# Fused attention and two mixture-of-experts layers on one core: the copies, low parts, ranks, slot gates and weight chunks between expert 7 and the fourth tile of the second layer change places

## The chip, the core and the metric

The kernel runs on one core of one Trainium2 chip. The time is the device time of one execution in microseconds; one program for each engine runs from the first attention block to the last scatter of the output. Shown are the median of three runs and one execution taken by the profiler. Engines are named as the profile names them: PE is TensorE, ACT ScalarE, DVE VectorE, POOL GpSimd, and SP the engine that issues the large loads.

## The reference

Windowed attention with sink tokens is followed by two mixture-of-experts layers. The first takes two experts for each token (noisy routing), the second one expert:

```python
def _moe2_ref(x, modality_id, w_gate, modality_bias, w1, w2):
    logits = x @ w_gate + modality_bias[modality_id]
    e_idx = np.argmax(logits, axis=1)
    probs = softmax(logits)                      # over the 8 experts
    gate_w = probs[np.arange(N), e_idx]
    for e in range(E):                           # E = 8, D = 512, F = 1024, N = 1536
        mask = e_idx == e
        h = np.maximum(x[mask] @ w1[e], 0.0)
        out[mask] = gate_w[mask, None] * (h @ w2[e])
```

The input x of this layer is the output of the first one. All values are float32; the kernel keeps that precision by splitting each operand of a product into a high part (rounded) and a low part (the rest), and adding three products: high by high, high by low, low by high.

## The kernel before

The program is written out by hand for each engine, and an engine executes its instructions in the written order. Semaphores alone tie the engines together, so the order in the text is the order on the chip. The first layer goes through eight experts, numbered 0 to 7. Expert 7 (`last` in the text) is its last. While it is computed, the router of the second layer already works on what the other experts have produced.

**What the second layer is made of.** The tokens are sorted by their expert and cut into tiles of 128 rows. The expert that most tokens of the first eight token blocks choose is called popular; its first two tiles (tiles 0 and 1) are made of tokens that are settled early, so that PE can begin while the rest of the routing is still under way. A tile t goes through these steps, which are small functions in the text:

- POOL `gather(t)` fetches its 128 rows from memory (L730); PE `tx(t)` turns them (L1320); ACT `x_high(t)` copies the turned rows as the high part (L1698) and DVE `x_low(t)` writes the low part (L2410).
- PE `first(t, half)` is the first product, in two halves of twelve 512-column matmuls: eight with the high part of the rows (L1339, L1340), four with the low part (L1344). ACT `relu(t, half)` copies the result (L1704).
- PE `th(t, half)` turns the hidden rows (L1354); ACT `h_high` (L1709) and DVE `h_low` (L2416) make their two parts.
- PE `second(t)` is the second product, again two halves of twelve matmuls (L1367, L1368, then L1371). DVE `y_copy(t)` scales the rows by their gates (L2424), and POOL scatters them.

From tile 4 on a loop runs these steps in a fixed pattern (`step`), in which `first` of tile t and `second` of tile t - 1 alternate.

**Weights.** A chunk is 128 by 2048 values, 1024 KB; an expert has four (0 and 1 for the first product, 2 and 3 for the second). SP loads it, ACT makes the high part, DVE the low part. Those of the popular expert are `popular_high(c)` (L1689) and `popular_low(c)` (L2402). Those of the expert that comes second in order are loaded by SP (L503 to L516) into `raw`, and converted by ACT and DVE in `second_weights` (L1446 and L1817); ACT's two calls of it stand between `x_high(2)` and `relu(2, 0)`, and behind `x_high(3)`. SP can load them only when it knows which expert it is: DVE's `expert_order()` (L2098 to L2106) says so.

**Routing of the second layer.** DVE `pick` finds each token's expert, PE `ranks(1)` counts (L956 to L960), DVE `second_places` (L2074 to L2090) finds each token's place, `second_hots` (L2093) and PE `codes2` (L977) make the list of rows that is gathered from tile 2 on, and `second_sources` (L2120 to L2126) writes it. ACT's exponential (L1766), DVE `chosen_gate` and POOL `coded_gates` (L709 to L718) lead to PE `slot_gates` (L1393) and DVE `slot_gates` (L2198 to L2201), the gates by slot, which every `y_copy` needs. `tile_owners` and `fresh_tiles` say which expert owns which tile.

**Expert 7.** PE's last product ends in `yT`; ACT `y1_copy(last, 3)` (L1592) takes its last part out of PSUM, and PE `last_logits(3)` (L1136) waits for that. PE `back(last, k)` (L1199) turns its rows back, four times, ACT `last_scale(k)` (L1624) scales them, and POOL scatters them. DVE `last_share` (L2333 to L2337) prepares its part in the router, which PE `last_to_tokens` (L1146) adds.

## Time and profile before

| | us |
|---|---|
| median of three runs | 679.68 |
| lowest and highest of the three | 679.19 and 680.46 |
| profiled execution | 680.44 |
| its span in the trace | 678.7 |
| PE busy | 640.8 (94%) |
| DVE busy | 328.6 (48%) |
| ACT busy | 275.7 (41%) |

The change lies between about 467 us, when PE ends the last product of expert 7, and 530.8 us, when the fourth tile's second product is still to come and the loop begins. Before and behind that stretch no instruction moves.

### The profile page before, as it was taken

How to read it: one execution, taken by the hardware profiler on the slowest of the kernel's cores; microseconds unless marked ns; L12 is line 12 of the kernel's file. 1: busy time of each engine (PE TensorE's matmuls, PEld its weight loads, DVE VectorE, ACT ScalarE, POOL GpSimd, SP SyncE). 2: the span in 40 equal slices, each digit the busy share in tenths (PEclk: the TensorE clock that was granted, in tenths of full speed). 3: DMA queues.
4: the chain of work that ended last, by engine and by line, in shares of the span. 5: the costliest groups of instructions: out<-in, count | busy, mean ns of one | idle time of the engine just before them, and what ended most of it. 6: DMA issues, size and time to landing. Idle time of an engine off the chain costs nothing.

```text
span 678.7 us, 11243 instructions
## 1 busy us (share of the span) xinstructions
PE 640.8 (94%) x3866; PEld 581.7 (86%) x3867; DVE 328.6 (48%) x681; ACT 275.7 (41%) x529; POOL 188.1 (28%) x199
## 2 busy tenths in 40 slices
PE   7989999899999999999999999998989999999981
PEld 6989999898999999999999998987767888788861
DVE  4466646586465527264452724566767222442220
ACT  5678866443344234243433523234516122522110
POOL 2500100127361633516153331101643122121010
PEclk9999999999999999999999999998989999999996
DMA  7878721354594546646364611515559311001000
GB/s 213 273 256 250 262 85 58 103 210 130 178 235 149 101 140 155 188 144 171 103 134 149 155 20 20 153 62 177 150 168 340 113 44 50 20 31 48 15 32 11
DMA packets 51089, 89.84 MB, mean 132 GB/s; under 512 B 7919, under 2 KB 14063, under 8 KB 51040
## 3 DMA queue, kind: packets, MB, share of 16 engines
q1 hardware_dynamic: 41872, 69.21, 30.8%
q0 software_dynamic: 9168, 19.97, 13.5%
q8 instruction: 31, 0.51, 0.3%
q14 instruction: 18, 0.15, 0.1%
HBM read 73.13 MB, written 17.02 MB: 133 GB/s over the span
## 4 chain that ended last, share of the span: by engine, by line
PE 80%; DVE 7%; DMA 4%; issue 3%; ACT 2%; SPq 1%; POOL 0%; ACTq 0%; DVEq 0%; POOLq 0%
PE banks L1058 6%; PE banks L1057 6%; PE banks L1076 6%; PE banks L996 5%; PE banks L997 5%; PE banks L999 5%; PE banks L801 5%; PE banks L829 4%; PE banks L1344 4%; PE banks L1339 4%; PE banks L1340 4%; PE banks L1367 3%; PE banks L1371 3%; PE banks L1368 3%; PE banks L813 2%
## 5 line engine op out<-in xcount | busy, mean ns | idle before, releaser
L1821 DVE TENSOR_TENSOR split<-stage,split 128x2048 fp32r<-128x2048 f32 x32 | 73.3, 2290 | 42.2 <-ACT split L1451 42.1
L996 PE MATMUL banks<-xTs,split 128*128 128x416 f32 (+1 forms) x256 | 88.7, 351 | 1.6 <-issue 1.6
L997 PE MATMUL banks<-xTs,split 128*128 128x416 f32 (+1 forms) x256 | 86.4, 342 | 0.0
L648 POOL DMA_INDIRECT x_moe<-rows,dst_idx x25 | 50.3, 2013 | 114.9 <-DVE rows L2271 112.9
L1057 PE MATMUL banks<-hTs,split 128*128 128x416 f32 x224 | 79.9, 357 | 0.0
L1058 PE MATMUL banks<-hTs,split 128*128 128x416 f32 x224 | 78.6, 351 | 0.0
L1586 ACT ACTIVATE hTs<-banks 128x416 fp32r<-128x416 f32 x56 | 29.0, 518 | 85.4 <-PE banks L999 85.4
L1451 ACT ACTIVATE split<-stage 128x2048 fp32r<-128x2048 f32 x32 | 60.9, 1908 | 0.5 <-DMA stage<-w1a 0.5
L1709 ACT ACTIVATE hTs<-banks 128x512 fp32r<-128x512 f32 x28 | 16.5, 598 | 105.1 <-PE banks L1354 105.1
L999 PE MATMUL banks<-xTs,split 128*128 128x416 f32 (+1 forms) x256 | 56.2, 341 | 0.0
L801 PE MATMUL banks<-k_sb,q_sb 128*128 128x260 f32 (+2 forms) x192 | 49.5, 384 | 3.4 <-DMA k_sb<-k_w 2.0
L1831 DVE CUSTOM_DVE_ANT_0 negs<-banks,masks 128x260 f32<-128x260 f32 (+2 forms) x96 | 35.0, 402 | 35.9 <-PE banks L801 34.5
L996 PEld LDWEIGHTS banks<-xTs,split 128*128 128x128 f32 x256 | 48.1, 188 | 2.5 <-issue 2.2
L1984 DVE SCALAR_TENSOR_TENSOR hTs<-banks,hTs 128x416 fp32r<-128x416 f32 x56 | 32.8, 587 | 35.8 <-ACT hTs L1586 35.7
L746 POOL DMA_INDIRECT out<-rows,dst x14 | 14.2, 1015 | 128.0 <-DVE rows L2424 118.5
L1464 ACT ACTIVATE probs<-negs,negmax 128x260 f32<-128x260 f32 (+2 forms) x96 | 46.1, 484 | 7.9 <-DVE negmax L1831 7.8
L1367 PE MATMUL banks<-split,hTs 128*128 (+1 forms) x112 | 45.7, 408 | 3.6 <-DVE rows L2424 1.8
L1339 PE MATMUL banks<-split,xTs 128*128 (+1 forms) x112 | 45.4, 405 | 3.6 <-issue 2.0
L2245 DVE TENSOR_TENSOR xTs<-banks,xTs 128x512 fp32r<-128x512 f32 (+1 forms) x28 | 16.6, 592 | 66.4 <-ACT xTs L1555 66.3
L997 PEld LDWEIGHTS banks<-xTs,split 128*128 128x128 f32 x256 | 48.2, 188 | 0.3
L1076 PE MATMUL banks<-hTs,split 128*128 128x416 f32 x224 | 48.0, 356 | 0.0
L999 PEld LDWEIGHTS banks<-xTs,split 128*128 128x128 f32 x256 | 46.3, 188 | 0.4
(371 smaller groups left out, 1313.6 us busy)
## 6 DMA issues: line engine op xcount, KB each, us to landing
stage<-w1a SPq DMA_DIRECT2D x16, 1024.0 KB, 7.3
stage<-w2a SPq DMA_DIRECT2D x16, 1024.0 KB, 5.5
k_sb<-k_w SPq DMA_DIRECT2D x12, 520.0 KB, 4.9
raw<-w1b SPq DMA_DIRECT2D x4, 1024.0 KB, 6.1
raw<-w2b SPq DMA_DIRECT2D x4, 1024.0 KB, 8.8
q_sb<-q_t SPq DMA_DIRECT2D x24, 128.0 KB, 4.1
x_attention<-rows SPq DMA_DIRECT2D x12, 256.0 KB, 6.0
split<-x_moe SPq DMA_DIRECT2D x12, 256.0 KB, 3.7
```

What stands on the lines that cost most here:

```text
L648: pool.indirect_dma_start(out=x_dram[1], out_offset=rows_at(dst_idx[0], early_dst, e, k), in_=y_lines(e, k), in_offset=None, compute_op=AL ...
L801: mm = pe.matmul(S[:, j % 2, h, 0:n], q_sb[:, b, pair, h, :], k_sb[:, b, pair, 0:n], start=True, stop=True)
L996: pe.matmul(psum, piece(slot, 0, o + c * FH), xTs[:, 0, c, 0:cols], start=(c == 0), stop=False)
L997: pe.matmul(psum, piece(slot, 1, o + c * FH), xTs[:, 0, c, 0:cols], start=False, stop=False)
L999: mm = pe.matmul(psum, piece(slot, 0, o + c * FH), xTs[:, 1, c, 0:cols], start=False, stop=(c == DC - 1))
L1057: pe.matmul(psum, piece(e % 2, 0, o), hTs[:, 0, c, 0:cols], start=(c == 0), stop=False)
L1058: pe.matmul(psum, piece(e % 2, 1, o), hTs[:, 0, c, 0:cols], start=False, stop=False)
L1076: mm = pe.matmul(psum, piece(e % 2, 0, DC * F + c * D + d * P), hTs[:, 1, c, 0:cols], start=False, stop=(c == FC - 1))
L1339: pe.matmul(psH[:, half, :], xTs2[:, 0, c, :], weights(slot, 0, o), start=(c == 0), stop=False)
L1367: pe.matmul(psY, hTs2[:, 0, c, :], weights(slot, 0, o), start=(c == 0), stop=False)
L1451: act.activation(split_chunk(e % 2, 0, c), staged_chunk(e % 2, c), ACT.Copy).then_inc(high_done[c], 1)
L1821: dve.tensor_tensor(split_chunk(e % 2, 1, c), staged_chunk(e % 2, c), split_chunk(e % 2, 0, c).bitcast(F32), ALU.subtract).then_inc(low_do ...
```

## The change

It changes the written order on four engines, and takes out one wait; no instruction with a result is added or taken away.

- ACT: `popular_high(0)` goes behind `y1_copy(last, 3)`. `relu(0, 0)` goes ahead of `last_scale(3)`, the exponential ahead of `relu(0, 1)`, `popular_high(3)` behind `x_high(1)`, and `parted_tiles` behind `h_high(0, 0)`.
- DVE: `popular_low(0)` goes behind `last_share`, `x_low(0)` and `popular_low(1)` ahead of `pick`. `chosen_gate` and `popular_low(2)` go ahead of `x_low(1)` and `second_places`. `h_low(0, 0)` and `popular_low(3)` go ahead of `second_sources`; `slot_gates` and `y_copy(0)` ahead of `expert_order`; `tile_owners` and `fresh_tiles` behind `h_low(1, 1)`; `y_copy(1)` ahead of the second expert's low parts.
- PE: `first(0, 0)` goes ahead of `back(last, 3)`, `ranks(1)` behind `tx(1)`. `codes2` moves into the middle of `second(0)`. The wait for all four `last_scale` moves from `first(0, 1)` to `th(0, 0)`; `first(0, 1)` waits for the first of them only. `th(2, 0)` goes ahead of `first(3, 0)`: the call of `step(3)` is written out for that.
- SP: ahead of the loads of the second expert's weights the wait for the gather of tile 2 is gone.

```diff
--- before.py
+++ after.py
@@ -508,7 +508,6 @@
             experts = sp.value_load(used[0:1, 1, 1:2], min_val=1, max_val=E)
             e = sp.value_load(order[0:1, 1:2], min_val=0, max_val=E - 1)
             sp.wait_ge(last_added, 1)
-            sp.wait_ge(gathered[0], 32)
             for c in range(CHUNKS):
                 if c == CHUNKS - 1:
                     sp.wait_ge(all_scattered, 1)
@@ -1358,8 +1357,11 @@
                     if not isinstance(t, int) or t > 0:
                         pe.wait_ge(y_copied, t)
                     for half in range(2):
-                        if isinstance(t, int) and t == 1 and half == 1:
-                            tx(2, 0, 2)
+                        if isinstance(t, int) and half == 1:
+                            if t == 0:
+                                codes2()
+                            elif t == 1:
+                                tx(2, 0, 2)
                         pe.wait_ge(low_done[2 + half], e + (E + 1))
                         pe.wait_ge(h_high_done, t * 2 + (half + 1))
                         for c in range(half * 4, half * 4 + 4):
@@ -1396,16 +1398,16 @@
 
                 tx(0, 0, 1)
                 back(last, 2, banks[:, 3, :])
+                first(0, 0, 0, 1)
                 back(last, 3, banks[:, 4, :])
-                first(0, 0, 0, 1)
-                ranks(1)
-                pe.wait_ge(scaled1, nth_sub(E, 0))
+                pe.wait_ge(scaled1, nth_sub(last, 0) + 1)
                 first(0, 1, 0, 1)
                 tx(1, 1, 1)
+                ranks(1)
                 first(1, 0, 0, 1)
+                pe.wait_ge(scaled1, nth_sub(E, 0))
                 th(0, 0)
                 first(1, 1, 0, 1)
-                codes2()
                 th(0, 1)
                 second(0, 0, 1)
                 slot_gates()
@@ -1413,11 +1415,17 @@
                 th(1, 1)
                 second(1, 0, 1)
                 pe.wait_ge(fresh_ready[1], 1)
-                e, slot = expert(2)
-                first(2, 0, e, slot)
-                first(2, 1, e, slot)
+                e2, slot2 = expert(2)
+                first(2, 0, e2, slot2)
+                first(2, 1, e2, slot2)
                 tx(3, 1, 2)
-                step(3, 1, 3)
+                th(2, 0)
+                e3, slot3 = expert(3)
+                first(3, 0, e3, slot3)
+                first(3, 1, e3, slot3)
+                th(2, 1)
+                tx(4, 0, 3)
+                second(2, e2, slot2)
                 with pe.Fori(2, sure // 2 - 1) as r:
                     step(r * 2, 0, r + 1)
                     step(r * 2 + 1, 1, r + 2)
@@ -1681,7 +1689,6 @@
                 y1_copy(last, 2)
                 x2_high(11)
                 turned_copy(2)
-                popular_high(0)
                 y1_copy(last, 3)
 
             def popular_high(c):
@@ -1752,22 +1759,23 @@
                             act.wait_ge(pe_route, 7)
                         high_part(1, c)
 
+                popular_high(0)
                 popular_high(1)
                 last_scale(0)
                 last_scale(1)
                 x_high(0)
                 last_scale(2)
+                relu(0, 0)
                 last_scale(3)
                 popular_high(2)
-                relu(0, 0)
-                popular_high(3)
-                relu(0, 1)
                 act.wait_ge(act_route, 6)
                 act.activation(rc[:], rb[:], ACT.Exp).then_inc(act_route, 1)
+                relu(0, 1)
                 x_high(1)
-                parted_tiles()
+                popular_high(3)
                 relu(1, 0)
                 h_high(0, 0)
+                parted_tiles()
                 relu(1, 1)
                 h_high(0, 1)
                 h_high(1, 0)
@@ -2456,36 +2464,36 @@
                         dve.wait_ge(high_done[c], E + 2)
                         low_part(1, c)
 
-                popular_low(0)
                 popular_first()
                 last_share()
-                popular_low(1)
+                popular_low(0)
                 late_scores()
                 all_scores()
+                x_low(0)
+                popular_low(1)
                 pick(noisy, 0, chosen[:], done_key)
                 dve.sem_inc(dve_route, 1)
                 link(dve.tensor_tensor(rb[:], noisy[:], over_e(top[:, 0, :]), ALU.subtract))
                 dve.sem_inc(act_route, 1)
-                x_low(0)
+                chosen_gate()
+                popular_low(2)
+                x_low(1)
                 second_places()
-                x_low(1)
-                chosen_gate()
                 second_hots()
-                popular_low(2)
-                second_sources()
                 h_low(0, 0)
                 popular_low(3)
+                second_sources()
                 h_low(0, 1)
+                slot_gates()
+                y_copy(0, 0, 0)
                 expert_order()
+                h_low(1, 0)
+                h_low(1, 1)
                 tile_owners()
                 fresh_tiles()
-                slot_gates()
-                y_copy(0, 0, 0)
-                h_low(1, 0)
-                h_low(1, 1)
                 x_low(2)
+                y_copy(1, 1, 0)
                 second_weights((0, 1))
-                y_copy(1, 1, 0)
                 x_low(3)
                 second_weights((2, 3))
                 next_weights(2)
```

On ACT at the end of expert 7 and in tile 0, before (`stage` are the staged weight chunks of the popular expert, `yT` the last part of expert 7's product, `raw` the scaled rows of expert 7):

```order
L1618 ACTIVATE rows<-banks 16x512
L1689 ACTIVATE split<-stage 128x2048
L1592 ACTIVATE yT<-banks 128x416
L1689 ACTIVATE split<-stage 128x2048
L1624 ACTIVATE raw<-banks,sub_gate 128x512 x2
L1698 ACTIVATE xTs<-banks 128x512
L1624 ACTIVATE raw<-banks,sub_gate 128x512 x2
L1689 ACTIVATE split<-stage 128x2048
L1704 ACTIVATE rows<-banks 128x512
L1689 ACTIVATE split<-stage 128x2048
L1704 ACTIVATE rows<-banks 128x512
L1766 ACTIVATE rc<-rb 128x96
```

and with the change, where the lines carry other numbers (L1592 is L1600, L1689 is L1696):

```order
L1626 ACTIVATE rows<-banks 16x512
L1600 ACTIVATE yT<-banks 128x416
L1696 ACTIVATE split<-stage 128x2048 x2
L1632 ACTIVATE raw<-banks,sub_gate 128x512 x2
L1705 ACTIVATE xTs<-banks 128x512
L1632 ACTIVATE raw<-banks,sub_gate 128x512
L1711 ACTIVATE rows<-banks 128x512
L1632 ACTIVATE raw<-banks,sub_gate 128x512
L1696 ACTIVATE split<-stage 128x2048
L1772 ACTIVATE rc<-rb 128x96
L1711 ACTIVATE rows<-banks 128x512
L1705 ACTIVATE xTs<-banks 128x512
```

The copy of `yT` no longer has the first weight chunk ahead of it, and the fourth weight chunk has gone behind the copy of tile 1's turned rows (`xTs`).

On DVE, from the low part of the hidden rows of tile 0 on, before (`used` and `order` are what the loads of the second expert wait for; the last row here is the first of `tile_owners`):

```order
L2402 TENSOR_TENSOR split<-stage,split 128x2048
L2416 TENSOR_TENSOR hTs<-banks,hTs 128x512
L2098 TENSOR_REDUCE noise_sb<-pair_up_to 128x2
L2099 CAST used<-noise_sb 128x1
L2101 TENSOR_TENSOR noise_sb<-pair,iota_row 128x8
L2102 SCALAR_TENSOR_TENSOR pair_sq<-iota_row,pair_up_to 128x64
L2103 TENSOR_TENSOR pair_sq<-pair_sq,noise_sb 128x64
L2104 TENSOR_REDUCE order_f<-pair_sq 128x8
L2105 CAST order<-order_f 128x7
L2110 SCALAR_TENSOR_TENSOR shared<-pair_up_to,iota_row 128x168
```

and with the change (`slot_gate` are the gates by slot, the row behind it is `y_copy(0)`):

```order
L2424 TENSOR_TENSOR hTs<-banks,hTs 128x512
L2206 COPY shared<-banks 128x63
L2208 TENSOR_TENSOR shared<-shared 128x21
L2209 TENSOR_TENSOR slot_gate<-shared 128x21
L2432 TENSOR_SCALAR rows<-banks,slot_gate 128x512
L2106 TENSOR_REDUCE noise_sb<-pair_up_to 128x2
L2107 CAST used<-noise_sb 128x1
L2109 TENSOR_TENSOR noise_sb<-pair,iota_row 128x8
L2110 SCALAR_TENSOR_TENSOR pair_sq<-iota_row,pair_up_to 128x64
L2111 TENSOR_TENSOR pair_sq<-pair_sq,noise_sb 128x64
L2112 TENSOR_REDUCE order_f<-pair_sq 128x8
L2113 CAST order<-order_f 128x7
```

Ahead of the order of the experts three instructions of the slot gates and the copy of tile 0's result have moved.

## Rows read from the trace of the kernel before

**Rows 1.** Windows: us, busy of PE, PEld, DVE, ACT, POOL, PEclk, DMA share, GB/s.
```profile
467.10:470.40 3.30, 1.50 (x15) 1.41 (x14) 1.13 (x1) 2.70 (x3) 2.00 (x2) 1.00 0.98 341
470.50:477.20 6.70, 6.14 (x73) 5.71 (x73) 6.13 (x16) 3.45 (x5) 3.11 (x1) 0.50 0.63 211
...
501.20:504.50 3.30, 1.48 (x10) 1.11 (x9) 2.94 (x11) 1.08 (x2) 0.02 (x1) 1.00 0.70 208
504.70:508.00 3.30, 3.30 (x9) 2.52 (x8) 0.05 (x1) 0.00 (x0) 0.80 (x1) 0.50 1.06 399
```

**Rows 2.** Timeline of PE: start, us, engine, line, operation, count, idle before and releaser.
```profile
469.69 1.20 PE L1136 MATMUL banks<-wg,yT 128*128 128x8 f32 x8 [1.80 <-ACT yT L1592]
...
473.88 1.44 PE L1146 MATMUL banks<-chosen,last_hot 128*128 128x24 bf16 x48 [0.56 <-DVEq L2338]
...
477.46 0.49 PE L1339 MATMUL banks<-split,xTs 128*128 128x512 f32 x1
...
480.21 1.21 PE L1344 MATMUL banks<-split,xTs 128*128 128x512 f32 x4 [0.64 <-DVE xTs L2410]
...
486.33 0.47 PE L1339 MATMUL banks<-split,xTs 128*128 128x512 f32 x1 [0.96 <-issue]
...
489.13 0.60 PE L1354 MATMUL banks<-ident,rows 128*128 128x128 f32 x4
...
497.47 0.50 PE L1367 MATMUL banks<-split,hTs 128*128 128x512 f32 x1 [1.00 <-DVE split L2402]
...
503.61 0.50 PE L1367 MATMUL banks<-split,hTs 128*128 128x512 f32 x1 [1.82 <-DVE rows L2424]
...
506.38 1.84 PE L1371 MATMUL banks<-split,hTs 128*128 128x512 f32 x4
...
510.35 1.07 PE L1371 MATMUL banks<-split,hTs 128*128 128x512 f32 x4
...
518.38 0.49 PE L1339 MATMUL banks<-split,xTs 128*128 x1 [1.08 <-issue]
...
530.79 0.39 PE L1339 MATMUL banks<-split,xTs 128*128 x1
```

**Rows 3.** Timeline of ACT, end of expert 7 to tile 2.
```profile
467.32 1.91 ACT L1689 ACTIVATE split<-stage 128x2048 fp32r<-128x2048 f32 x1 [1.40 <-DMA stage<-w1b]
469.14 0.50 ACT L1592 ACTIVATE yT<-banks 128x416 f32<-128x416 f32 x1
470.01 1.91 ACT L1689 ACTIVATE split<-stage 128x2048 fp32r<-128x2048 f32 x1 [0.37 <-DMA stage<-w1b]
...
477.15 1.28 ACT L1624 ACTIVATE raw<-banks,sub_gate 128x512 f32<-128x512 f32 x2 [0.26 <-PE banks L1199]
...
509.19 3.71 ACT L1446 ACTIVATE split<-raw 128x2048 fp32r<-128x2048 f32 x2
```

**Rows 4.** Timeline of DVE, same stretch.
```profile
472.60 0.19 DVE L2333 TENSOR_TENSOR counts<-banks,sub_gate 128x32 f32<-128x32 f32 x1
...
487.73 1.77 DVE L2093 TENSOR_TENSOR row_hot<-row_i,iota_row 128x1536 bf16<-128x1536 int32 x1 [0.15 <-DVE gate L2237]
...
497.93 0.16 DVE L2098 TENSOR_REDUCE noise_sb<-pair_up_to 128x2 f32<-128x16 f32 x1
...
502.11 0.23 DVE L2198 COPY shared<-banks 128x63 f32<-128x63 f32 x1
...
511.13 4.49 DVE L1817 TENSOR_TENSOR split<-raw,split 128x2048 fp32r<-128x2048 f32 x2 [1.11 <-ACT split L1446]
```

**Rows 5.** Timeline of SP: first loads of the second expert.
```profile
500.97 0.93 SPq L362 DMA_DIRECT2D raw<-w1b  x2
```

**Rows 6.** Source line of those loads, chunks 0 and 1: us from issue to landing.
```profile
DMA to landing us min/median/max: 5.1/6.8/8.6
```

**Rows 7.** The same for chunks 2 and 3.
```profile
DMA to landing us min/median/max: 11.4/12.7/14.1
```

**Rows 8.** Timeline of POOL in the gates by slot.
```profile
485.31 0.61 POOL L606 TENSOR_TENSOR moving<-xT,code 128x252 bf16<-128x252 f32 x1 [2.22 <-DVEq L2090]
...
487.98 1.60 POOL L713 TENSOR_TENSOR gate_rest<-gate,gate_parts 128x12 f32<-128x12 f32 x1
...
492.38 1.75 POOL L718 TENSOR_TENSOR moving_gate<-xT,gate_parts 128x252 bf16<-128x252 f32 x3
```

## The prediction

> **What bounds the kernel now.** I read the profile's page first: PE is busy 640.8 of 678.7 us, and nothing outside 467 to 531 us is moved, so the question is what PE loses in that stretch. The timeline of PE shows it as waits of 1.80 us for ACT's copy of the last part of expert 7's product, 0.56 us for DVE's `last_share`, 0.64 us for `x_low(0)`, 0.96 us for `x_high(1)`, 1.00 us for the low part of weight chunk 3, 1.82 us for `y_copy(0)`, and 1.08 us ahead of `first(3, 0)` [rows 2], seven waits and 7.86 us in all. The windows show a second loss. The granted clock is at its lower level, 1.2 GHz, from about 470.5 to 477.2 us and from about 504.7 to 508.0 us. In the 3.3 us ahead of the first fall PE was busy 1.50 us, in the 3.3 us ahead of the second 1.48 us [rows 1]. What that costs stands in the timeline: the half of `second(1)` with the fall in it starts at 503.61 us, its last four matmuls take 1.84 us, the last four of the other half 1.07 us [rows 2]. The whole slow half lasts 1.6 us longer than a half at 2.4 GHz (twelve matmuls, 2.7 to 2.9 us).
>
> My measure of the change is the start of `first(4, 0)`, the loop's first matmul, at 530.79 us [rows 2]. Behind it nothing is changed, so what it moves by, the end moves by.
>
> **The change part by part.** I follow PE through the stretch and put the rows in their new order.
>
> *End of expert 7.* ACT's first weight chunk waited for its DMA until 467.32 us and ran 1.91 us, and the copy of `yT` stood behind it, at 469.14 [rows 3]. Now the copy comes first, at about 467.3, and PE's wait of 1.80 us goes. What is late next is ACT: the second chunk can't start before its DMA lands, at 470.01 as before. From there 1.86 us for the chunk (half of the pair at 3.71), 1.28 us for two `last_scale` and 0.6 us for `x_high(0)` [rows 3] give 473.8 us for `first(0, 0)`. It started at 477.46 [rows 2]: 3.7 us earlier. DVE is ready by then: `last_share` takes 1.3 us (472.60 to 473.88, where PE went on) [rows 2, 4] and now starts at about 469.1, `popular_low(0)` takes 2.25 us behind it (half of 4.49), so it ends near 472.7. `last_to_tokens` then starts at about 470.4, its 0.56 us of wait gone as well; neither is on the path, since ACT is later.
>
> *Tiles 0 and 1, first product.* From `first(0, 0)` to `th(0, 0)` PE took 11.67 us, 477.46 to 489.13. The waits of 0.64 and 0.96 us go: `x_low(0)` no longer stands behind `pick`, and the ranks now lie between `tx(1)` and `first(1, 0)` and cover most of `x_high(1)`. A new one comes: `popular_low(2)` now stands ahead of `x_low(1)` on DVE, 2.25 us, and the low part of `first(1, 0)` waits for it; with the eight matmuls ahead of it as cover I get 0.9 us, and 0.1 us is left of the wait for `x_high(1)`. `th(0, 0)` starts at 473.8 + 11.67 - 1.6 + 1.0 = 484.9, 4.2 us earlier. The bounds of the new wait are nothing and the whole 2.25 us.
>
> *Tile 0, second product.* Up to its second half 8.34 us (489.13 to 497.47). The wait of 1.00 us falls to 0.5: chunk 3 is converted behind `x_high(1)`, but PE comes earlier too. About 0.3 us for `h_low(0, 0)` behind `second_sources` goes. The second half starts at 492.4, 5.1 us earlier. From there to `second(1)` 6.14 us, 1.82 of them wait. `slot_gates` no longer has the order of the experts and the tile owners ahead of it (497.93 to 502.11 us [rows 4]), but it still follows PE's own `slot_gates` matmuls, so its 1.5 us (502.11 to 503.61) stay partly uncovered: two `th` of 0.45 us lie beside it, 0.9 us is left, and 0.5 us is for `h_low(0, 1)` behind `popular_low(3)` and `second_sources`. `second(1)` starts at 492.4 + 6.14 - 1.82 + 1.4 = 498.1, 5.5 us earlier.
>
> *Tile 1.* 503.61 to 511.26 us held 1.6 us of low clock. The wait of 1.82 us ahead of the fall is halved, and I take it that the fall goes. The order of the experts now stands ahead of `h_low(1, 0)`, 1.75 us, and leaves PE 0.55 us of wait. So `first(2, 0)` starts at 498.1 + 7.65 - 1.6 + 0.55 = 504.7, 6.5 us earlier.
>
> *Where it is given back.* The weights of the second expert do not come earlier. DVE starts `expert_order` at 497.93 us [rows 4] and SP issues the first load at 500.97 [rows 5], 3.04 us later. In the new order it follows `y_copy(0)`, which ends as `second(1)` starts: 498.1, so the first load is at 501.1. The wait that SP loses (the gather of tile 2, issued near 494.5) is over by then in either kernel: worth nothing, with these two times 3 us apart. Chunk 1 is issued 0.5 us later and lands 8.6 us after that [rows 6], at 510.2. ACT has its conversion ahead of `relu(2, 0)`; before, the chunks found ACT ready at 509.19 with both halves of the pair run through at once [rows 3]. Now ACT is there at about 503, waits, and is done at 510.2 + 1.9 = 512.1, and `relu(2, 0)` ends at 512.7. `th(2, 0)`, now ahead of `first(3, 0)`, is ready on PE at about 510.7 and starts at 512.8: 2.1 us of new wait. Behind it `relu(2, 1)` and `x_high(3)` put `first(3, 0)` at 513.8, where before it was at 518.38. The 12.41 us from there to `first(4, 0)` lose the 0.36 us of `th(2, 0)`. That gives 525.8: 5.0 us earlier, not 6.5. PE's queue is the only one held here. DVE's conversion of the same chunks stands ahead of `x_low(3)`, which is needed only 1.8 us after `first(3, 0)` starts. Chunk 3 lands 14.1 us after its issue [rows 7], near 516.7, and its conversion ends near 518.6 on ACT and 520.9 on DVE, just ahead of what `second(2)` needs.
>
> *The clock.* The fall at 470.5 I expect again, since PE is no busier with wide work ahead of it (turns and 8-column products). Whether the clock is back when `first(0, 0)` starts at 473.8, and whether it falls after the new wait of 2.1 + 0.6 us near 512, I can't read from a trace. Each costs 1.6 us by the row of `second(1)` [rows 2]. I count one of them: 5.0 - 1.6 = 3.4 us. Bounds: none, 5.0 us; both, 1.8 us.
>
> *The sum.* 680.44 us is the profiled execution's own time (span 678.7). Less 3.4 it is 677.0. The median of three runs is 0.76 us lower than that execution; less 3.4 from the median is 676.3. I say 676.6.
>
> **The rivals.**
>
> *No stretch of low clock is added* (5.0 us faster, 675.1 by the same mean of the two references). For it: before, the clock came back with PE busy 6.14 of 6.70 us [rows 1], and the new order packs the same work. Against: two separate places must go well.
>
> *POOL holds the slot gates.* From the one-hot table (485.31 us) to the end of its last product (492.38 + 1.75) POOL took 8.8 us, of which 1.8 waited for the gate. In the new order the table is ready at about 487.4, so POOL ends near 494.5, and PE asks for it at about 495.6. But `row_hot` now follows the table at once. Before, a subtraction of 12 elements a row on POOL, started at 487.98, took 1.60 us and ended as DVE's `row_hot` (487.73, 1.77 us) did [rows 4, 8]. If the 0.61 us product of POOL is held in the same way, POOL is 1.8 us later, 0.7 us behind PE, and the time is 677.3. The Trainium skill, GPSIMD Engine Reference, section Specifications, says that GpSimd shares its SBUF interfaces with VectorE and meets contention from VectorE instructions with two SBUF inputs; the rows agree, and by that rule this rival is the one that comes.
>
> *The loads land later.* If chunk 1 lands as chunk 2 did, after 11.4 us [rows 7], `th(2, 0)` waits 2.8 us more; with the one stretch of low clock 0.6 us are left of the gain, 679.4. For it: all four chunks are in flight at once, and the output's scatter now runs beside them.
>
> *Slower.* One mechanism: ACT stands in its queue at chunk 1 of the second expert, with `relu(2, 0)` behind it. If the four loads share the engines so evenly that chunk 1 lands with the last, after 14.1 us [rows 7], `th(2, 0)` is 5.5 us later: 3.4 - 5.5 = 2.1 us slower, 682.1. It decides from a landing of 8.6 + 3.4 = 12.0 us on. Against: the four landed in order, 5.1, 8.6, 11.4 and 14.1 us after their issues [rows 6, 7].
>
> **How the numbers follow.** Forecast 0.57, no added low clock 0.18, POOL 0.09, later loads 0.11, slower 0.05. What a measurement of this kernel can tell from no change is about 0.2%, 1.36 us: under 678.3 is faster. The first three cases are faster, 0.84; the later loads are mostly within 0.2%, 0.11; slower 0.05. The range runs from the rival without low clock by the median (679.68 - 5.0 = 674.7) to both stretches counted against the profiled execution (680.44 - 1.8 = 678.6), which takes in most of what lies between forecast and later loads: 674.8 to 678.9.
>
> **What would show it.** Right: the copy of `yT` ahead of the first chunk and `first(0, 0)` near 473.8 us; `second(1)` near 498; the first load of the second expert still near 501; ACT waiting for a DMA ahead of L1446's line, and a wait of about 2 us on PE ahead of `th(2, 0)`, which was not there. Wrong: `first(2, 0)` no earlier than 508, or `th(2, 0)` without a wait (then the gain is nearer 6 us), or a fall of the clock in more than two places.

## The result, and the profile after

| | before | after |
|---|---|---|
| median, us | 680.34 (20 runs, 677.79 to 682.43) | 676.3 (20 runs, 675.13 to 680.94) |
| profiled execution | 680.44 | 676.85 |
| its span | 678.7 | 674.9 |

The ratio is 0.9942, 95% interval 0.9928 to 0.9956: the changed kernel is faster, by 4.0 us in the medians. 676.6 us was predicted.

The page after: PE is busy 1.8 us less than before, with as many instructions; its share of the span is 95%.

```profile
span 674.9 us, 11238 instructions
...
PE 639.0 (95%) x3866; PEld 580.0 (86%) x3867; DVE 329.6 (49%) x681; ACT 275.7 (41%) x529; POOL 185.5 (27%) x199
```

Nothing is changed ahead of the last eight matmuls of expert 7, yet they start at 467.02 us in this profile and at 465.36 in that of before. Times that I call shifted have these 1.66 us taken off, so that they compare with those of the prediction; all others are as the trace has them. Seven of the eleven other profiles below have this point between 466.6 and 467.7 us and the rest later, so it is the profile of before that was early. It is also why the two profiled executions differ by only 3.6 us, less than the stretch below. The timeline of PE after, with the same steps as in [rows 2] (line numbers are one lower up to L1353, L1367 is L1369, L1371 is L1373, `slot_gates` is L1395):

```profile
468.61 1.85 PE L1135 MATMUL banks<-wg,yT 128*128 128x8 f32 x16
...
472.00 1.35 PE L1145 MATMUL banks<-chosen,last_hot 128*128 128x24 bf16 x48 [0.17 <-DVEq L2346]
...
475.27 0.47 PE L1338 MATMUL banks<-split,xTs 128*128 128x512 f32 x1 [0.99 <-ACT xTs L1705]
...
482.73 0.47 PE L1338 MATMUL banks<-split,xTs 128*128 128x512 f32 x1 [0.19 <-issue]
...
485.51 1.19 PE L1343 MATMUL banks<-split,xTs 128*128 128x512 f32 x4 [0.71 <-DVE xTs L2418]
486.54 0.60 PE L1353 MATMUL banks<-ident,rows 128*128 128x128 f32 x4
...
494.22 0.50 PE L1369 MATMUL banks<-split,hTs 128*128 128x512 f32 x1 [0.69 <-DVE split L2410]
...
496.98 1.21 PE L1373 MATMUL banks<-split,hTs 128*128 128x512 f32 x4 [0.64 <-DVE hTs L2424]
...
500.13 0.50 PE L1369 MATMUL banks<-split,hTs 128*128 128x512 f32 x1 [0.63 <-DVE rows L2432]
...
502.52 1.20 PE L1373 MATMUL banks<-split,hTs 128*128 128x512 f32 x4 [0.28 <-DVE hTs L2424]
...
506.77 0.39 PE L1338 MATMUL banks<-split,xTs 128*128 x1
...
514.01 0.66 PE L1353 MATMUL banks<-ident,rows 128*128 128x128 f32 x4 [1.18 <-ACT rows L1711]
515.33 0.50 PE L1338 MATMUL banks<-split,xTs 128*128 x1 [0.66 <-ACT xTs L1705]
...
527.25 0.39 PE L1338 MATMUL banks<-split,xTs 128*128 x1
```

The reader is to see two things. The wait of 1.80 us for `yT` is gone, and the one of 1.82 us for `y_copy(0)` is 0.63 us. And there are ten waits where there were seven: 6.14 us against 7.86, only 1.72 us less. The new ones are those of 0.99, 0.71, 0.64, 0.28, 1.18 and 0.66 us. The last two stand ahead of `th(2, 0)` and `first(3, 0)`.

`first(4, 0)` starts 60.23 us behind the last matmuls of expert 7, before 65.43: 5.20 us less. So 3.5 of the 5.2 us are not waits: PE went through the same work faster, at the higher clock. What of that is a gain by itself is tested further down (filled waits). Windows of after (columns as in [rows 1]), where the first fall was and around the new wait:

```profile
467.00:475.20 8.20, 7.10 (x99) 6.60 (x95) 5.88 (x19) 6.54 (x8) 2.26 (x3) 1.00 0.76 253
...
512.90:516.00 3.10, 1.33 (x7) 1.02 (x8) 2.49 (x2) 3.10 (x5) 2.11 (x2) 1.00 1.04 405
```

The granted clock stays at 2.4 GHz through the whole stretch. Before, PE was at 1.2 GHz for 6.8 and 3.4 us of it [rows 1].

ACT after, the rows that answer to [rows 3] (L1592 is L1600, L1689 is L1696, L1624 is L1632, L1698 is L1705, L1704 is L1711, L1446 is L1454):

```profile
468.80 0.52 ACT L1600 ACTIVATE yT<-banks 128x416 f32<-128x416 f32 x1 [1.21 <-PE banks L1075]
469.22 1.90 ACT L1696 ACTIVATE split<-stage 128x2048 fp32r<-128x2048 f32 x1
471.57 1.91 ACT L1696 ACTIVATE split<-stage 128x2048 fp32r<-128x2048 f32 x1 [0.45 <-DMA stage<-w1b]
473.39 1.25 ACT L1632 ACTIVATE raw<-banks,sub_gate 128x512 f32<-128x512 f32 x2
474.53 0.60 ACT L1705 ACTIVATE xTs<-banks 128x512 fp32r<-128x512 f32 x1
...
508.18 1.92 ACT L1454 ACTIVATE split<-raw 128x2048 fp32r<-128x2048 f32 x1 [3.38 <-DMA raw<-w1b]
511.56 1.92 ACT L1454 ACTIVATE split<-raw 128x2048 fp32r<-128x2048 f32 x1 [1.47 <-DMA raw<-w1b]
513.38 1.07 ACT L1711 ACTIVATE rows<-banks 128x512 f32<-128x512 f32 x2
```

The copy of `yT` now waits for PE alone, and chunk, two scalings and the copy of the turned rows follow each other to `first(0, 0)`. At the second expert's chunks ACT waits for the DMA, 3.38 and 1.47 us, where before it ran both at once; `relu(2, 0)` (L1711) comes when the second is done, and PE 0.6 us behind its start.

DVE after, the rows that answer to [rows 4] (L2093 is L2101, L2402 is L2410, L2198 is L2206, L2098 is L2106):

```profile
488.91 2.22 DVE L2101 TENSOR_TENSOR row_hot<-row_i,iota_row 128x1536 bf16<-128x1536 int32 x1
...
491.89 2.28 DVE L2410 TENSOR_TENSOR split<-stage,split 128x2048 fp32r<-128x2048 f32 x1
...
498.63 0.23 DVE L2206 COPY shared<-banks 128x63 f32<-128x63 f32 x1 [1.70 <-PE banks L1395]
...
499.99 0.16 DVE L2106 TENSOR_REDUCE noise_sb<-pair_up_to 128x2 f32<-128x16 f32 x1
```

POOL in the gates by slot ([rows 8]; L606 is L605, L718 is L717):

```profile
488.91 0.61 POOL L605 TENSOR_TENSOR moving<-xT,code 128x252 bf16<-128x252 f32 x1 [5.61 <-DVEq L2098]
489.47 1.71 POOL L708 CAST gate_parts<-gate 128x12 bf16<-128x12 f32 x1
...
492.08 2.13 POOL L714 CAST gate_parts<-gate_rest 128x12 bf16<-128x12 f32 x1
494.30 1.75 POOL L717 TENSOR_TENSOR moving_gate<-xT,gate_parts 128x252 bf16<-128x252 f32 x3
```

And the first load of the second expert ([rows 5]), with the times from issue to landing of its chunks 0 and 1 and of chunks 2 and 3 ([rows 6, 7]):

```profile
502.98 0.93 SPq L362 DMA_DIRECT2D raw<-w1b  x2
...
DMA to landing us min/median/max: 5.2/6.6/8.0
...
DMA to landing us min/median/max: 10.8/11.9/12.9
```

It is issued 35.96 us behind the last matmuls of expert 7 (before: 35.61 us). All that PE gained ahead of it did not make it earlier.

### The profile page after: what moved, and what is told of

Its sections match the earlier page's. It is cut to its first block, busy times and chain, and to the rows that moved or that the text cites. A ratio compares the mean times of both kernels' runs of the same rounds, so it can differ in the third digit from the quotient of the medians.

```text
span 674.9 us, 11238 instructions
## 1 busy us (share of the span) xinstructions
PE 639.0 (95%) x3866; PEld 580.0 (86%) x3867; DVE 329.6 (49%) x681; ACT 275.7 (41%) x529; POOL 185.5 (27%) x199
## 4 chain that ended last, share of the span: by engine, by line
PE 80%; DVE 7%; DMA 4%; issue 3%; ACT 3%; SPq 1%; ACTq 0%; POOL 0%; DVEq 0%; POOLq 0%
PE banks L1057 6%; PE banks L1056 6%; PE banks L1075 6%; PE banks L996 5%; PE banks L995 5%; PE banks L998 5%; PE banks L800 5%; PE banks L828 4%; PE banks L1373 3%; PE banks L1338 3%; PE banks L1343 3%; PE banks L1339 3%; PE banks L1369 3%; PE banks L1370 3%; PE banks L812 2%
## 5 line engine op out<-in xcount | busy, mean ns | idle before, releaser
L1369 PE MATMUL banks<-split,hTs 128*128 (+1 forms) x112 | 45.3, 404 | 2.1 <-ACT hTs L1716 0.7
```

The costliest lines, as they stand in the source:

```text
L1369: pe.matmul(psY, hTs2[:, 0, c, :], weights(slot, 0, o), start=(c == 0), stop=False)
```

## The experiments

In each profile I read the stretch from the start of expert 7's last matmuls to `tx(5)`, PE's turn of tile 5's rows (L1319 or L1320). It is 71.79 us before and 66.60 us after. Stretch and waits come from one execution each, ratios from all runs. The profiled execution is not always a typical one: of the kernels with `relu(2)` first, with order first and low parts too, and with SP's wait back it was the slowest of six or seven. The first four kernels ran on one chip, on which the kernel before took 681.15 us, the next four on a second (680.57), the last three on a third (685.36). Medians compare within a chip only.

| kernel | median, us | ratio to before, 95% | stretch, us |
|---|---|---|---|
| the change, run again | 677.78 | 0.9945 [0.9926, 0.9963] | 68.02 |
| end of expert 7 alone | 679.32 | 0.9988 [0.9962, 1.0013] | 68.86 |
| expert order first | 675.62 | 0.9920 [0.9892, 0.9948] | 65.01 |
| `relu(2)` first | 676.46 | 0.9921 [0.9892, 0.9949] | 65.61 |
| order first, low parts too | 676.87 | 0.9942 [0.9921, 0.9964] | 65.09 |
| SP's wait back | 675.77 | 0.9930 [0.9912, 0.9949] | 68.01 |
| gates last | 677.87 | 0.9978 [0.9957, 0.9999] | 67.04 |
| chunk 1 third | 681.48 | 1.0017 [0.9999, 1.0034] | 70.95 |
| filled, before | 687.41 | 1.0025 [0.9990, 1.0060] | 70.58 |
| filled, after | 683.49 | 0.9961 [0.9928, 0.9995] | 66.69 |
| order and `relu(2)` first | 683.12 | 0.9952 [0.9917, 0.9987] | 65.44 |

**The change, run again.** No edit.

> The change itself, as the mark for the other kernels here. My theory (the part worked out in the prediction: waits of PE go at six places, and one comes back ahead of th(2, 0) since ACT waits for the second expert's chunk 1): 3.4 to 5 us faster than before, ratio 0.993 to 0.995, with PE's wait ahead of th(2, 0) at 1 to 2.5 us. Rival, that the gain is the granted clock alone: the ratio goes to 0.997 to 1.000 in runs where the kernel before happens to keep its clock.

The stretch was 1.42 us longer than in the first profile of the same kernel. Its timeline of PE, and its windows:

```profile
514.40 0.66 PE L1353 MATMUL banks<-ident,rows 128*128 128x128 f32 x4 [1.06 <-ACT rows L1711]
```

```profile
512.90:516.50 3.60, 1.88 (x12) 1.30 (x11) 2.61 (x2) 3.38 (x5) 2.11 (x2) 1.00 1.03 397
516.80:520.00 3.20, 3.20 (x9) 2.52 (x8) 2.29 (x1) 2.54 (x3) 0.45 (x2) 0.50 1.05 391
```

Here the clock fell to 1.2 GHz from 516.7 to 520.1 us, behind the waits of 1.06 and 0.66 us. It fell in the first half of `first(3, 0)`, which has twelve wide matmuls, so all of it is lost (I take the 1.42 us for its cost). The stretch of low clock that the forecast counted is thus something that this kernel does in one execution and not in the next. The rival, that the gain is the clock alone, falls by the mean granted clocks of the executions: at the same 0.984, 0.985 and 0.987 the change (five executions) is still 2.0 to 3.2 us faster than the kernel before (fourteen).

**The end of expert 7 alone**, in the kernel before:

```diff
@@ ACT @@
                 turned_copy(2)
-                popular_high(0)
                 y1_copy(last, 3)
...
+                popular_high(0)
                 popular_high(1)
@@ DVE @@
-                popular_low(0)
                 popular_first()
                 last_share()
+                popular_low(0)
                 popular_low(1)
```

> The kernel before with the end of expert 7 alone changed: the copy of yT ahead of the first weight chunk on ACT, and last_share ahead of popular_low(0) on DVE. By my theory first(0, 0) starts 3 us earlier, but x_low(0) still stands behind pick on DVE, so the low matmuls of first(0, 0) wait about 2 us and only 1.7 us are kept: ratio about 0.9975, the other waits as before. Rival A, that this end is the whole gain of the change: 4 us faster, 0.994. Rival B, that the start of the second layer is bound by something else (a DMA): no gain, 1.000.

The turn of tile 0 came 3.6 us earlier, the turn of tile 1 only 1.35 us. Between them, in the timeline of PE:

```profile
480.33 1.19 PE L1344 MATMUL banks<-split,xTs 128*128 128x512 f32 x4 [2.46 <-DVE xTs L2410]
```

The wait for `x_low(0)`, 0.64 us before [rows 2], is 2.46 us: the time gained is lost again behind `pick`. The waits behind it are as before. The stretch is 2.93 us shorter, but this execution lacks the fall at 504.6 us, worth 1.6 us; 1.3 us are the edit's. In the runs it can't be told from no change. The forecast had counted on 1.7 us and a ratio of 0.9975. So one of the two longest waits of the profile (1.80 us), removed alone, gives less than its own length, since the next queue takes the rest.

**Expert order first**, in the changed kernel, on DVE:

```diff
                 h_low(0, 1)
+                expert_order()
                 slot_gates()
                 y_copy(0, 0, 0)
-                expert_order()
                 h_low(1, 0)
```

> The change, with expert_order put ahead of slot_gates on DVE, where DVE idles 1.70 us for PE. Theory (PE's wait ahead of th(2, 0) is the landing of the second expert's chunk 1, held up by the order of the experts): SP's first load is issued 3 us earlier, PE's waits of 1.18 and 0.66 us there go, and so does the 0.28 us for h_low(1, 0): 2 us faster than the change, ratio to before about 0.991. Rival, that ACT's own conversions, whenever the data come, hold relu(2, 0): the wait stays, ratio as the change's.

SP's first load, two rows of PE, and ACT's conversion of chunk 1:

```profile
499.71 0.93 SPq L362 DMA_DIRECT2D raw<-w1b  x2
```

```profile
500.00 0.50 PE L1369 MATMUL banks<-split,hTs 128*128 128x512 f32 x1 [0.75 <-DVE rows L2432]
...
512.29 0.66 PE L1353 MATMUL banks<-ident,rows 128*128 128x128 f32 x4
```

```profile
509.84 1.92 ACT L1454 ACTIVATE split<-raw 128x2048 fp32r<-128x2048 f32 x1 [2.19 <-DMA raw<-w1b]
```

The load comes 3.2 us earlier, `th(2, 0)` has no wait of note, and `second(1)` waits 0.12 us more. The stretch is 1.59 us shorter than after, where 2 us were expected. Two things kept the rest. Chunk 1 landed 9.5 us after its issue instead of 8.0, so it came 1.66 us earlier and not 3.2, and ACT still waited 2.19 us for it: the landing still sets when `relu(2, 0)` runs. And the wait ahead of `first(3, 0)`, 0.66 us after, did not go as expected but was 0.74 us. Why the chunk took longer was not tried. `expert_order` (499.99 to 501.63 us after) fits in DVE's idle 1.70 us ahead of the gates, the row at 498.63 above. This is what I had overlooked: in the change these seven small instructions stand behind a wait which they could have filled.

**`relu(2)` first**, in the changed kernel, on ACT and in the same way on DVE:

```diff
-                second_weights((0, 1))
+                second_weights((0,))
                 relu(2, 0)
...
                 x_high(3)
-                second_weights((2, 3))
+                second_weights((1, 2, 3))
```

> The change, with only chunk 0 of the second expert converted ahead of relu(2, 0) on ACT (chunks 1 to 3 behind x_high(3)), and DVE's low parts in the same order. The loads come no earlier. Theory (ACT's queue holds relu(2, 0) behind chunk 1's landing): the waits of 1.18 and 0.66 us ahead of th(2, 0) and first(3, 0) go, but chunk 3 is converted as late as before, so h_low(2, 0) makes second(2) wait some 0.7 us: about 1.1 us faster than the change, ratio to before 0.992 to 0.993. Rival, that the wait is DVE's or PE's own: no difference to the change.

The timeline of PE:

```profile
513.85 0.49 PE L1338 MATMUL banks<-split,xTs 128*128 x1 [0.64 <-issue]
...
522.64 1.20 PE L1373 MATMUL banks<-split,hTs 128*128 x4 [0.33 <-DVE hTs L2424]
```

The wait ahead of `th(2, 0)` is gone with the loads issued no earlier; 0.33 us come back in `second(2)`. The stretch is 0.99 us shorter. The 0.66 us ahead of `first(3, 0)`, expected to go as well, stayed (0.64). DVE's order was changed along with ACT's, so it is the trace that tells the two apart: in the change ACT waits 1.47 us for chunk 1 with `relu(2, 0)` next in its queue, and PE's releaser is that `relu`.

**Order first, low parts too.** The kernel with `expert_order` first, and `x_low(1)` ahead of `popular_low(2)`, `h_low(0, 1)` ahead of `second_sources`:

```diff
                 chosen_gate()
-                popular_low(2)
                 x_low(1)
+                popular_low(2)
...
                 popular_low(3)
-                second_sources()
                 h_low(0, 1)
+                second_sources()
```

> x2_order_first, and two more exchanges on DVE: x_low(1) ahead of popular_low(2), and h_low(0, 1) ahead of second_sources. Theory (the short waits of PE left at these two places are DVE's order, with nothing behind them): the waits of 0.54 us ahead of first(1, 0)'s low matmuls and of 0.64 us ahead of second(0)'s go, 1.2 us faster than x2, ratio to before about 0.990. Rival: the places or the list of rows come later for it, and PE waits for the slot gates or the gather of tile 2 instead: no faster than x2.

The timeline of PE (this profile is 4.5 us late before the stretch begins):

```profile
504.26 0.50 PE L1369 MATMUL banks<-split,hTs 128*128 128x512 f32 x1 [1.20 <-DVE rows L2432]
...
517.04 0.66 PE L1353 MATMUL banks<-ident,rows 128*128 128x128 f32 x4 [0.66 <-ACT rows L1711]
```

The two waits I aimed at (0.54 and 0.64 us in the kernel with `expert_order` first) are gone, and the stretch was to shrink by 1.2 us. It was 65.09 us against 65.01: the expectation fell. The waits stand elsewhere: 0.90 us for `h_low(0, 0)`, 1.20 us for the gates and 0.66 us ahead of `th(2, 0)`. Between `x_low(1)` and `y_copy(0)` DVE's own chain (two low parts of 2.3 us, the places, the one-hot rows, the sources) is what ends last: it runs without a listed wait from 487.08 to 504.12 us in this trace, and the order inside it only chooses where PE stands still.

**SP's wait back**, in the changed kernel:

```diff
             sp.wait_ge(last_added, 1)
+            sp.wait_ge(gathered[0], 32)
```

> The change with SP's wait for the gather of tile 2 put back ahead of the second expert's loads. Theory (the gather has landed 2 us before the order of the experts is known): first load at the same time, ratio as the change's, 0.994 to 0.995. Rival (the wait's removal brings the loads forward and is part of the gain): 1 us or more slower than the change.

SP's first load:

```profile
503.33 0.93 SPq L362 DMA_DIRECT2D raw<-w1b  x2
```

That is 35.89 us behind the last matmuls of expert 7 (467.44 us here), 35.96 without the wait. Taking it out was worth nothing there, and the runs don't show a gain either (0.9930 with it, 0.9942 and 0.9945 without). The stretch is 1.4 us longer since the clock fell at 515.7 us, behind the same pair of waits as in the second run of the change. It fell once more at 471.3 us, as in the kernel with `expert_order` first at about 471.1 us, for 3.4 us each time; `first(0, 0)` started 8.38 and 8.29 us behind the last matmuls of expert 7, against 8.04 to 8.25 us in the seven profiles of this order without one. There it cost 0.3 us at most.

**Gates last**, in the changed kernel: `expert_order`, `tile_owners` and `fresh_tiles` back ahead of `slot_gates` and `y_copy(0)`.

```diff
                 h_low(0, 1)
+                expert_order()
+                tile_owners()
+                fresh_tiles()
                 slot_gates()
                 y_copy(0, 0, 0)
-                expert_order()
                 h_low(1, 0)
                 h_low(1, 1)
-                tile_owners()
-                fresh_tiles()
```

> The change with DVE's expert_order, tile_owners and fresh_tiles back ahead of slot_gates and y_copy(0). Theory: y_copy(0) and second(1) come 2.2 us later than in the change, but the second expert's loads are issued 3 us earlier, so the waits of 1.2 and 0.6 us ahead of th(2, 0) and first(3, 0) go nearly whole, and the end hardly moves against the change (0 to 0.5 us slower, and up to 1.6 us more where the granted clock falls behind the longer wait). Rival (the exchange on DVE carries the gain): 2 us or more slower than the change in the stretch from expert 7's last matmuls to tile 4.

```profile
502.23 0.50 PE L1369 MATMUL banks<-split,hTs 128*128 128x512 f32 x1 [3.17 <-DVE rows L2432]
```

PE waits 3.17 us for `y_copy(0)` instead of 0.63 (the row above is of PE's timeline). The turn of tile 2 is 1.88 us later than after, the turn of tile 4 only 0.44 us: `th(2, 0)` waits no longer, since the loads are earlier. Only 0.4 of 2.5 us is left in the profile. The runs say more: 2.1 us above the kernel with SP's wait, on the same chip. A fall of the clock behind the long wait in some executions would do a part of it. This profile shows none, but its mean granted clock, 0.992, is the highest of its twelve executions; the three executions that had it took 676.9 us, the nine at 0.982 to 0.990 took 677.5 to 684.5. Even those three are about 1 us above the one execution with SP's wait at 0.993, so the rest stays open.

**Chunk 1 third**, in the changed kernel: SP loads the second expert's chunks in another order.

```diff
-            for c in range(CHUNKS):
+            for c in (0, 2, 1, 3):
```

> The change with SP loading the second expert's chunks in the order 0, 2, 1, 3, so that chunk 1 lands third. Nothing else is moved. Theory (the landing of chunk 1 starts th(2, 0), through ACT's queue): PE's wait ahead of th(2, 0) grows from 1.2 to about 4.5 us, 3.4 us slower than the change, ratio to before 0.998 to 1.001. Rival (ACT or DVE work is what th(2, 0) waits for, and the landing is hidden): ratio as the change's.

The timeline of PE and that of ACT:

```profile
517.01 0.98 PE L1353 MATMUL banks<-ident,rows 128*128 128x128 f32 x4 [4.88 <-ACT rows L1711]
```

```profile
514.56 1.91 ACT L1454 ACTIVATE split<-raw 128x2048 fp32r<-128x2048 f32 x1 [5.13 <-DMA raw<-w1b]
```

With chunk 1 later, the wait ahead of `th(2, 0)` is 4.88 us instead of 1.18, and the clock falls behind it (mean granted 0.51 from 517.1 to 520.5 us). The stretch is 4.35 us longer than after, and in the runs the whole gain of the change is gone. This is the mechanism of the slower rival, made to happen. It did not in the change because the chunks land one after the other, as before.

**Filled waits.** To price the clock by itself, products of 512 columns with ones into unused banks were added: sixteen to the kernel before (ahead of its waits of 1.80 and 1.82 us), nine to the changed kernel.

```diff
@@ before @@
             last_logits(2)
+            keep_clock_up(8, banks[:, 4, :])
             last_logits(3)
...
                 th(1, 1)
+                keep_clock_up(8, psX)
                 second(1, 0, 1)
@@ after @@
+                keep_clock_up(3, banks[:, 4, :])
                 first(0, 0, 0, 1)
...
+                keep_clock_up(6, banks[:, 2, :])
                 th(2, 0)
```

> The kernel before with two of PE's waits filled: eight products of 512 columns with ones (their results are overwritten, nothing of the output changes) ahead of last_logits(3), where PE waited 1.80 us, and eight between th(1, 1) and second(1), where it waited 1.82 us. The waits themselves stay. It prices the granted clock apart from the waits. Theory: of the 5.2 us between the two profiled executions 3.5 us are time at the lower clock in the kernel before and only 1.7 us waits, so with the falls gone the kernel before gets 1.5 to 3.5 us faster, ratio 0.995 to 0.998. Rival (the falls are mere company of the waits, and the change gains by its waits): no change, 1.000.

> The change with its two longest waits of PE filled in the same way: three products ahead of first(0, 0) and six ahead of th(2, 0). Theory: the changed kernel still loses 1.4 us in executions whose clock falls behind the wait at th(2, 0), so filled it is 0 to 1 us faster than the change, ratio to before 0.992 to 0.994. Rival (the clock has nothing left to give there): as the change; if the products run at the lower clock ahead of first(0, 0) they cost up to 0.4 us.

The kernel before with filled waits had one fall (483.4 to 486.8 us) instead of 6.8 and 3.4 us of low clock, and was only 1.21 us shorter in the stretch. Its timeline of PE:

```profile
483.57 1.44 PE L1146 MATMUL banks<-chosen,last_hot 128*128 128x24 bf16 x48 [1.75 <-DVEq L2340]
...
496.67 0.47 PE L1340 MATMUL banks<-split,xTs 128*128 128x512 f32 x1 [1.62 <-issue]
```

The waits for `last_share` and for `x_high(1)` were 0.56 and 0.96 us [rows 2] and are 1.75 and 1.62 us. `second(1)` started 38.57 us behind the last matmuls of expert 7, before 38.25: with 3.4 us less at 1.2 GHz nothing was gained up to there, the time given back became waits for DVE and ACT. Behind it, where the second fall had been, `tx(2)` followed 2.87 us later instead of 4.45: those 1.6 us came back whole, as they did in the kernel with the end of expert 7 alone (2.88 us). So of the 3.5 us that are not waits, 1.6 us are a gain by themselves. The other 1.9 us belong to the 6.8 us of the first fall. Half of these were taken away here and gave nothing: they lay beside work of DVE and ACT that PE, in the old order, would have waited for anyway. The other half was not tested.

In the runs it gained nothing, where 0.995 to 0.998 was expected. That says little of the clock's worth, since the filling hardly raised it: the mean granted clock is 0.983 over its twelve executions and 0.983 over those of the kernel before on that chip. The filled changed kernel has a fall of 3.4 us of its own (at 479.0 us) and tells nothing: 66.69 against 66.60 us. The change itself was not run on that chip.

**Order and `relu(2)` first**, both edits in the changed kernel.

> x2_order_first and x3_relu_first together: expert_order ahead of slot_gates on DVE, and chunks 1 to 3 of the second expert converted behind x_high(3). Theory: x2 alone already takes the landing out of PE's way, so the two gains don't add: stretch from expert 7's last matmuls to tile 4 as in x2 (about 1.6 us shorter than the change's), ratio to before 0.991 to 0.992. Rival: they add (2.6 us shorter), 0.990.

```profile
518.83 0.49 PE L1338 MATMUL banks<-split,xTs 128*128 x1 [0.64 <-issue]
```

65.44 us, against 65.01 and 65.61 with one of them. The gains do not add: both take away the same wait of 1.18 us, and the 0.6 us ahead of `first(3, 0)` (row above, PE's timeline) stay for `x_high(3)`. The ratio is above the 0.991 to 0.992 expected, though its interval reaches there. The kernel with `expert_order` first has the shortest stretch that I found; in the runs it can't be told from the one with `relu(2)` first. Its interval overlaps that of the change on the same chip; its median is 2.2 us lower, of which 1.6 us show in the stretch.

## Why the prediction was right

By its own steps, in shifted times:

| step | predicted | measured |
|---|---|---|
| `first(0, 0)` | 473.8 | 473.6 |
| `th(0, 0)` | 484.9 | 484.9 |
| second half of `second(0)` | 492.4 | 492.6 |
| `second(1)` | 498.1 | 498.5 |
| first load of the second expert | 501.1 | 501.3 |
| `first(2, 0)` | 504.7 | 505.1 |
| `th(2, 0)` | 512.8 | 512.4 |
| `first(3, 0)` | 513.8 | 513.7 |
| `first(4, 0)` | 525.8 | 525.6 |

*End of expert 7: right.* `first(0, 0)` was 3.85 us earlier where 3.7 was computed, by ACT's chain from the landing of the second chunk. What the prediction did not say is that the 3.7 us depend on the rest: alone they came to 1.3 us. The fall of the clock at 470.5 us, which it expected again, did not come in this profile. It came in two other profiles of this order and cost 0.3 us at most.

*The new waits: right in place, small errors in size.* For `x_low(1)` 0.9 us were given and 0.71 measured; 0.1 and 0.19 for `x_high(1)`; 0.5 and 0.69 for chunk 3; 0.5 and 0.64 for `h_low(0, 1)`; 0.9 and 0.63 for the gates; 0.55 and 0.28 for `h_low(1, 0)`.

*POOL: the rival fell, since its delay was already in the sum.* POOL took 7.1 us from the table (488.91) to the end of its last product (494.30 + 1.75), as computed, and ended 2.0 us ahead of PE's own `slot_gates` at 498.04; DVE then waited 1.70 us for PE. The two engines did hold each other up, but with two long instructions on POOL as before, which the 7.1 us hold already, and not with a third. The product of 0.61 us and DVE's `row_hot` started at the same moment, and it was `row_hot` that grew, from 1.77 [rows 4] to 2.22 us; the product kept its 0.61. POOL's next instruction, of 12 elements a row, took 1.71 us and ended with `row_hot`, and a later one 2.13 us, as long as DVE's low part at 491.89. The same kind of instruction took 0.19 us when DVE's instruction did not have two inputs in SBUF (the second CAST, between them, in this trace). The rule that the prediction cited beside this rival gives no direction. The Trainium skill, SBUF — State Buffer, section "SBUF: two separate sides", says that the pair of ports which the two engines share goes for a whole instruction to the one that starts first; these rows agree in which of the two was held, though `row_hot` grew by 0.45 us and not by the product's 0.61. By that rule it is the order of starts, not the kind of instruction alone, that says which of the two pays.

*The loads: right.* They stay at `y_copy(0)`'s end, and the wait that SP lost was worth nothing in time of issue (the run with it back: 35.89 against 35.96 us). Chunk 1 landed 8.0 us after its issue where 8.6 was used.

*The give-back: right in place, 0.9 us too large.* 2.1 us were predicted ahead of `th(2, 0)`, 1.18 measured. PE was there 0.5 us later than computed, and chunk 1 landed 0.3 us earlier. Three kernels bear the mechanism out: chunk 1 late makes the wait 4.88 us; loads issued earlier, or `relu(2, 0)` ahead of the chunk, remove it. The wait of 0.66 us behind it, ahead of `first(3, 0)`, is `x_high(3)`, as computed.

*The clock: the term that can't be had from one profile.* The forecast counted one more stretch of low clock, 1.6 us. The profile after has none, so its gain in the stretch, 5.20 us, is the first rival's 5.0. The second profile of the same kernel has one, at the place named ahead (behind the wait near 512 us), for 1.42 us; so has the kernel with SP's wait back. Of the kernel before there is one profile only; but the kernel with the end of expert 7 alone, which has the old order at that place and a wait of 1.78 us there, lacks the fall at 504.6 us. So low clock in this stretch comes and goes in the changed kernel from one execution to the next, and it seems to in the old one. The medians differ by 4.04 us, by the ratio's interval 3.0 to 4.9 us. That lies between the forecast's 3.4 and the rival's 5.0. For every execution the mean granted clock is known, though not where it was low. On the chip of the second run it is 0.9835 over 22 of before and 0.9871 over 11 of the change. Over a span of 677 us that is an estimated 5 us less at 1.2 GHz (0.0036 x 677 / 0.5, since the clock is halved there), where the two profiled executions differ by 10.2. The pair of profiles thus shows about twice the usual difference in clock, which is in line with 4.0 us in the medians and 5.2 in the profiles. How many executions had a fall at which place it can't tell. That the number came out within 0.3 us also owes something to the reference: the forecast was made from an execution that was 1.66 us early at its point of departure and took the same time in all, so its own stretch was longer than is usual by about as much. In that part the number is luck. The range was not drawn as it was worked out either: its bounds come to 674.7 and 678.6 us, and 674.8 to 678.9 is what is stated.

## What to carry to other kernels

A wait that is removed is worth what the next queue behind it lets through: follow the bounding engine to a point where nothing moves any more, and price each new wait on the way. Here ten waits took the place of seven, and the stretch still became 5.2 us shorter. When a chain of one engine binds, exchanging steps inside it moves the waits of the others about and gains nothing; a gain comes from putting a step into that engine's own idle time, as with the seven small instructions ahead of the gates, since SP's loads hang on them. And a time at low clock is not to be added to the waits as if it were free to take back: first ask whether another engine would have held PE for as long. Here one fall was worth its whole 1.6 us, and the half of the other that was taken away nothing.

## What the runs showed of the hardware

- One and the same kernel had PE's clock fall behind waits of 1.06 and 0.66 us in one execution (3.4 us at 1.2 GHz, 1.42 us lost), and not behind waits of 1.18 and 0.66 us in another.
- Time at 1.2 GHz cost 1.6 us of 3.3 where PE had wide matmuls and nothing else to wait for, and nothing where ACT and DVE ended later anyway: 3.4 us less of it left `second(1)` 0.3 us later.
- With DVE working on two inputs in SBUF, a POOL instruction of 12 elements a row took 1.71 and 2.13 us instead of 0.19 us. In return a DVE instruction that started with POOL's product took 2.22 us instead of 1.77 (2.21 or 2.22 in all ten profiles with the new order, 1.77 in all three with the old).
- Four loads of 1024 KB in flight together landed 5.2, 8.0, 10.8 and 12.9 us after their issues. Issued 3.2 us earlier, the first two took 6.0 and 9.5 us. Chunk 3 of the popular expert landed 11.1 us after its issue, where before it took 7.6 us; why was not tried. ACT waited 2.95 us for it and PE nothing, since DVE's chain was later anyway:

```profile
485.58 1.92 ACT L1696 ACTIVATE split<-stage 128x2048 fp32r<-128x2048 f32 x1 [2.95 <-DMA stage<-w2b]
```
